# Second batch's probabilities transposed once: GpSimd adds the two blocks of a head, two triangles of ones part them again

## What is computed

```python
keep = (pos[None, :] < 4) | ((rel >= 0) & (rel < 128))   # rel = query - key
scores = np.where(keep, q @ k.T / 8, -1e9)
a = softmax(scores)
x = (a @ v) with the heads side by side                  # (2, 768, 512)
# mixer 1: low-rank token mixing (rank 32), then 512 -> 2048 -> 512
u = x + (x.T @ U @ V).T;           x = u + relu(u @ w1) @ w2
# mixer 2: 768 -> 256 -> 768 over the tokens, then 512 -> 1536 -> 512
u = x + (relu(x.T @ t1) @ t2).T;   out = u + relu(u @ w1) @ w2
```

## Time and profile before

| | us |
|---|---|
| median of three runs | 650.76 |
| profiled execution | 652.52 |
| its span | 650.7 |
| TensorE busy, matmuls | 632.9 |
| VectorE / ScalarE / GpSimd busy | 337.0 / 318.3 / 370.1 |

### The profile page before, as it was taken

One profiled execution on the slowest core, in us unless ns is written; L12 is line 12 of the kernel. 1 busy time (PEld: TensorE's weight loads), 2 busy tenths in 40 slices (PEclk: granted clock), 3 DMA queues, 4 the chain that ended last, 5 costly groups with the idle time before them and its releaser, 6 DMA issues.

```text
span 650.7 us, 10398 instructions
## 1 busy us (share of the span) xinstructions
PE 632.9 (97%) x3554; PEld 568.0 (87%) x3554; DVE 337.0 (52%) x720; ACT 318.3 (49%) x723; POOL 370.1 (57%) x371
## 2 busy tenths in 40 slices
PE   8999899999999999999999999999999999999997
PEld 6889698988989997999999988899998888899986
DVE  7776543332333422657576652297568226675411
ACT  5667644545544453745445444555445446344321
POOL 8545445655646473475757563585756446657262
PEclk9999989999999999999999999999999999999999
DMA  7434144342334242233222333233233343421142
GB/s 174 109 80 129 37 128 118 99 126 81 98 92 152 69 130 80 81 96 114 77 102 81 114 93 101 83 112 113 67 114 98 102 141 98 131 97 34 49 141 86
DMA packets 88420, 65.51 MB, mean 101 GB/s; under 512 B 43024, under 2 KB 72464, under 8 KB 88368
## 3 DMA queue, kind: packets, MB, share of 16 engines
q1 hardware_dynamic: 88368, 64.85, 35.1%
HBM read 61.42 MB, written 3.15 MB: 99 GB/s over the span
## 4 chain that ended last, share of the span: by engine, by line
PE 87%; DVE 5%; issue 3%; ACT 3%; POOL 1%; DMA 0%; DVEq 0%; ACTq 0%; POOLq 0%
PE bank L1400 34%; PE bank L1190 22%; PE bank L1366 10%; PE bank L1256 4%; PE bank L1227 4%; PE bank L1330 3%; PE bank L1293 3%; PE bank L1235 2%; PE bank L1307 2%; PE bank L1210 1%; PE bank L1274 1%; DVE masked L984 1%; PE bank L1392 1%; POOL w_lo L770 1%; DVE k_hi L962 1%
## 5 line engine op out<-in xcount | busy, mean ns | idle before, releaser
L770 POOL TENSOR_TENSOR w_lo<-w_raw,w_hi 128x512 fp32r<-128x512 f32 (+1 forms) x158 | 208.9, 1329 | 158.2 <-ACT w_hi L791 157.8
L791 ACT ACTIVATE w_hi<-w_raw 128x512 fp32r<-128x512 f32 (+1 forms) x158 | 96.5, 618 | 60.9 <-PE bank L1400 42.2
L1190 PE MATMUL bank<-b_hi,a_hi 128*128 128x384 f32 x280 | 94.6, 338 | 1.5 <-DVE temps L1096 1.5
L1190 PE MATMUL bank<-b_lo,a_hi 128*128 128x384 f32 x280 | 94.8, 339 | 0.0
L1400 PE MATMUL bank<-w_hi,hid_hi 128*128 128x512 f32 x216 | 87.6, 405 | 0.0
L1400 PE MATMUL bank<-w_hi,hid_lo 128*128 128x512 f32 x216 | 85.1, 394 | 0.0
L1400 PE MATMUL bank<-w_lo,hid_hi 128*128 128x512 f32 x216 | 84.7, 392 | 0.0
L823 ACT ACTIVATE probs<-masked,neg_max 128x264 f32<-128x264 f32 x96 | 49.5, 516 | 64.8 <-DVE neg_max L984 64.4
L1400 PE MATMUL bank<-w_hi,y_hid 128*128 128x512 f32 x216 | 71.1, 395 | 0.2
L984 DVE CUSTOM_DVE_ANT_0 masked<-bank,masks 128x264 f32<-128x264 f32 x96 | 41.1, 430 | 46.2 <-PE bank L1227 43.0
L735 POOL COPY p_sink<-probs 128x12 f32<-128x12 f32 x96 | 19.4, 204 | 72.1 <-ACT probs L823 70.7
(11 more groups left out here) (143 smaller groups left out, 1418.1 us busy)
## 6 DMA issues: line engine op xcount, KB each, us to landing
w_raw<-in_moe_w_ch_dram SPq DMA_DIRECT2D x144, 256.0 KB, 2.7
w_raw<-in_moe_w_ch_dram SPq DMA_DIRECT2D x20, 512.0 KB, 3.5
q_nat<-in_q_dram SPq DMA_DIRECT2D x12, 256.0 KB, 3.0
k_nat<-in_k_dram SPq DMA_DIRECT2D x12, 256.0 KB, 3.6
v_nat<-in_v_dram SPq DMA_DIRECT2D x12, 256.0 KB, 4.0
out_dram<-o_stage SPq DMA_DIRECT2D x11, 256.0 KB, 3.3
w_raw<-in_moe_w_tok_dram SPq DMA_DIRECT2D x6, 256.0 KB, 2.7
w_raw<-in_moe_w_tok_dram SPq DMA_DIRECT2D x8, 192.0 KB, 2.3
```

The lines of the kernel that those rows point to most:

```text
L770: nc.gpsimd.tensor_tensor(w_lo[:, split % NW, 0:n], w_raw[:, split % NR, 0:n], w_hi[:, split % NW, 0:n].bitcast(f32), ALU.subtract) \
L791: nc.scalar.activation(w_hi[:, split % NW, 0:n], w_raw[:, split % NR, 0:n], ACT.Copy) \
L1190: last = mm(bank[:, 0:HALF], w[at % 2][:, a, k, :], u[:, b_part, k, :], start=(first and n == 0), stop=(n == 5), skip_group_check=True)
```

## The change

For T = 7 to 11, the tiles of the second batch with two blocks: GpSimd adds the previous block's probabilities onto the own block's (one 128x128 sum for each head, ahead of its sink copy), TensorE waits for that sum and transposes it once, and VectorE, for all heads, multiplies the transposed sum from PSUM by two triangles of ones (key <= query, key > query) into the two halves of `probs_T`. The products with v stay. The triangles are built once by GpSimd in a part of `o_stage`, at the step `pv` of u = 8.

```diff
+        triangles = o_stage[:, 2, 0:2 * P].rearrange("p (a b) -> p a b", a=2)
...
         def blocks(T):
+            if T > NQ:
+                return [(0, T), (0, T - 1)]
...
+        def two_triangles(T):
+            return T > NQ
+
         def by_act(u):
-            return u % 2 == 1
+            return u % 2 == 1 and not two_triangles(u // H)
+
+        def act_copies(u):
+            return sum(by_act(v) for v in range(u + 1))
...
             elif by_act(at):
-                eng.wait_ge(probsT_by_act, (at + 1) // 2)
+                eng.wait_ge(probsT_by_act, act_copies(at))
             else:
-                eng.wait_ge(probsT_by_dve, at + 1 - (at + 1) // 2)
+                eng.wait_ge(probsT_by_dve, at + 1 - act_copies(at))
... (GpSimd)
                     copied += 1
+                    if two_triangles(T):
+                        pool.wait_ge(probs_ready, u + 1)
+                        nc.gpsimd.tensor_tensor(probs[:, u % 4, 0:P], probs[:, u % 4, 0:P],
+                                                probs[:, u % 4, BLK:BLK + P], ALU.add).then_inc(blocks_added, 1)
...
+                elif s == ("pv", H):
+                    nc.gpsimd.memset(triangles[:, :, :], 1.0).then_inc(triangles_built, 1)
+                    pool.wait_ge(triangles_built, 1)
+                    for n, step in enumerate((1, -1)):
+                        part = triangles[:, n, :]
+                        nc.gpsimd.affine_select(out=part, in_=part, compare_op=ALU.is_ge, fill=0.0, base=-n,
+                                                pattern=[[step, P]], channel_multiplier=-step) \
+                          .then_inc(triangles_built, 1)
... (VectorE)
-                    nc.vector.tensor_copy(probs_T[:, u % 2, 0:n], tp_banks[tp_bank_of[s]][:, 0:n]) \
-                      .then_inc(probsT_by_dve, 1)
+                    transposed = tp_banks[tp_bank_of[s]]
+                    if two_triangles(u // H):
+                        dve.wait_ge(triangles_built, 3)
+                        nc.vector.tensor_tensor(probs_T[:, u % 2, :].rearrange("p (a b) -> p a b", a=2),
+                                                transposed[:, 0:P].unsqueeze(1).broadcast_to([P, 2, P]),
+                                                triangles[:, :, :], ALU.mult).then_inc(probsT_by_dve, 1)
+                    else:
+                        nc.vector.tensor_copy(probs_T[:, u % 2, 0:n], transposed[:, 0:n]).then_inc(probsT_by_dve, 1)
... (TensorE)
                     tp_free(s)
-                    for j, (col, _) in enumerate(blocks(u // H)):
+                    if two_triangles(u // H):
+                        pe.wait_ge(blocks_added, u - (NQ + 1) * H + 1)
+                    for j, (col, _) in enumerate(blocks(u // H)[0:1 if two_triangles(u // H) else 2]):
```

More of the change, by code:

```diff
@@ L390, in attention_then_two_mixers @@
         masks_built = sem("masks_built")
+        triangles_built = sem("triangles_built")
+        blocks_added = sem("blocks_added")
         khi_zeroed = sem("khi_zeroed")
```

## The result

The changed kernel took 647.44 us (median of four, 646.91 to 648.74) against 650.78 us: a ratio of 0.9951, 95% interval 0.9938 to 0.9964, so 0.49% faster where 0.57% was forecast. A second set of runs gave 647.18 us, 0.9945 (0.9932 to 0.9958). Among the experiments, one execution of e5 was disturbed (1575 us) and is left out of its ratio.

The account below looks back on a forecast made before the run. TensorE, busy 97% of the 650.7 us span, was taken to bound the kernel. Savings of 32 x 0.11 + 4 x 0.04 + 4 x 0 = 3.7 us off the 650.76 us median gave 647.1 us, range 645.9 to 649.0.

Parts of the forecast that it names:

- The transposes, on the path: Units of T = 7 to 11: one transpose less on TensorE saves 0.11 us, in 32 units.
- Four sink stalls swallow the gain: Last heads of T = 7 to 10: the sink transpose waits for VectorE's masking, so these four units win nothing.
- Four units out of a stall earn 0.04 us: Units whose transposes start after a stall, three behind q's drain, one behind k: 0.04 us won each.
- GpSimd's sum and its queue: zero: Forty added 128x128 sums on GpSimd, 0.53 us each, and the work queued behind them cost TensorE nothing.
- GpSimd sets the pace: Rival, 7%: adds stretched to 1.5 us fill GpSimd's time per unit; gain gone, about 650.7 us.
- Part of the gain: Rival, 7%: adds arrive late in 12 of 40 units where GpSimd also splits q or k; 648.4 us.
- The added wait costs TensorE: Rival, 8%: a third wait before each of 40 transposes costs 0.15 us, 6.0 us in all; slower, 653.1 us.
- VectorE's multiply: zero: Copy out of PSUM as a 128x256 multiply, 0.43 us, one SBUF input: no collision with GpSimd, no cost.
- The triangles: zero: GpSimd's memset and two affine_selects behind the sink copy at 24.4 us: 1.4 us of work, covered, no cost.

Follow-up runs that it names:

- e5: Changed kernel with two spare GpSimd sums ahead of the real one in each of the 40 units; 652.34 us, ratio 1.0012.
- e1: Kernel before plus GpSimd's sum, written to a spare place, and TensorE's wait for it, still two transposes; 650.88 us, ratio 0.9998.
- e2: Kernel before with VectorE making all copies of transposed probabilities for T = 7 to 11; 650.93 us, ratio 1.0001.
- e3: Changed kernel without GpSimd's sum and TensorE's wait, so the output omits the previous block's probabilities; 647.61 us, ratio 0.9948.
- e8: Changed kernel with the sink transpose issued after six matmuls of the following mixer piece, T = 6 to 10; 642.77 us, ratio 0.9874.
- e9: Kernel before, two transposes kept, with the sink transpose issued inside the following mixer piece; 646.81 us, ratio 0.9935.

## Why the prediction was right

- *The transposes, on the path.* Forecast 0.11 us a unit, read from T = 6. Right: away from the stalls the units gained 0.09 to 0.13 us each (one, u = 64, only 0.03), and e1, e2 and e3 leave nothing else that could have made the gain.
- *Four sink stalls swallow the gain.* Right: the spacing of 1.01 us there did not move, and e8 against e9 gives the missing 0.46 us back once the stalls are gone.
- *Four units out of a stall earn 0.04 us.* Right behind the transpose (0.13 for 0.16), but incomplete: the stalls themselves became shorter, by 0.04 to 0.05 us each (0.59 for 0.63 at q's drain), which the forecast didn't have. That makes 0.2 us in all, and the sum came out at 3.7 partly because the other units gained a little less than 0.11 on average.
- *GpSimd's sum and its queue: zero.* Right; e1 shows it. The size was 0.48 where 0.53 was taken.
- *GpSimd sets the pace*, the rival, with 650.7 us from sums of 1.5 us. The real sum took 0.48, so it did not come about. e5 tried its price: three sums, 1.4 us of work, gave the kernel before's time within 0.2%. The number was right, and GpSimd's average room was indeed nearly gone. But TensorE did not wait in every unit: two thirds of the loss fell on the single unit in which GpSimd is late anyway.
- *Part of the gain*, the rival of 648.4 us with sums late in 12 units: TensorE waited for none of the sums.
- *The added wait costs TensorE*, the slower rival: excluded by e1.
- *VectorE's multiply: zero*, 0.42 us with one SBUF input beside GpSimd's work, 414 to 425 ns over all 40, and 414 to 426 in e5, where GpSimd is busy 95% of the time. Right. The rule cited from the Trainium skill, GPSIMD Engine Reference, Key points, is borne out: one SBUF input, no collision.
- *The triangles: zero.* Right: up to T = 6 both profiles keep step.
- The median fell by 3.3 us where 3.7 were forecast, within its interval; the stretch and the profiled pair, which have less noise, say 3.7 and 3.8.

## What to carry to other kernels

A unit of the kernel that already does what the edit will do elsewhere (here T = 6) prices the edit better than any duration: the spacing said 0.11 us where the duration said 0.28. Count such a saving only in units whose end TensorE sets itself; just before a wait for another engine it is worth nothing, until that wait is gone. And the room for added work on a helper engine is the room at its worst place in the queue, not its average idle time: one more sum in each unit already cost 0.4 us there while 16.6 us of waiting were left elsewhere.

## What was not expected of the hardware

**A dip of the clock, and a late start.** Executions of the kernel before differ by up to 1.9 us. The stretch tables from 81 to 86 us, the changed kernel first and then its second profile:

```profile
81.00:86.00 5.00, 4.74 (x24) 4.61 (x25) 2.20 (x7) 2.10 (x7) 1.41 (x2) 0.66 1.10 272
```
```profile
81.00:86.00 5.00, 4.69 (x33) 4.56 (x34) 3.60 (x11) 2.43 (x8) 1.42 (x2) 1.00 1.09 277
```

The granted clock is 0.66 in one and 1.00 in the other, a fall to the lower of its two levels (1.2 for 2.4 GHz) for most of it; twelve transposes take 2.77 us in one and 1.47 in the other, and everything behind comes 1.5 us later. In front of it TensorE was busy for only 2.6 of 4 us (77 to 81), in both. The first profile of the kernel before has the dip too, so that pair compares fairly, but medians mix executions with and without it.

There is a second source. In the profile of e3 no clock is lowered between 77 and 87 us, and yet its T = 7 begins 1.3 us later than in the second profile of the changed kernel. The difference is there from the first score product on (that second profile first, then e3):

```profile
7.16 0.60 PE L1241 MATMUL bank<-ident,q_nat 128*128 128x128 f32 x4
...
8.61 0.36 PE L1258 MATMUL bank<-k_hi,q_hi 128*128 128x264 f32 x1 [0.41 <-DVE k_lo L510]
```
```profile
8.32 1.06 PE L1237 MATMUL bank<-ident,q_nat 128*128 128x128 f32 x4
...
9.89 0.57 PE L1254 MATMUL bank<-k_hi,q_hi 128*128 128x264 f32 x1
```

Both lie before the edit does anything. Why TensorE is slower there for longer is open.

**One sum and one wait more, a shorter stall.** At q's drain the transpose starts 0.58 to 0.60 us after the product with v in the kernels in which GpSimd makes its sum in time and a third, long satisfied wait for it stands before the transpose, and 0.63 to 0.64 us in those without (the kernel before, e2, e3, e9). The timelines of e1, with two transposes, and e3, with one:

```profile
126.38 0.55 PE L1266 MATMUL bank<-v_nat,probs_T 128*128 128x64 f32 x4
...
126.97 0.41 PE L1245 MATMUL bank<-ident,probs 128*128 128x128 f32 x2
```
```profile
127.30 0.55 PE L1283 MATMUL bank<-v_nat,probs_T 128*128 128x64 f32 x4
...
127.93 0.30 PE L1262 MATMUL bank<-ident,probs 128*128 128x128 f32 x1
```

Three such stalls lie in the stretch, about half of e3's 0.26 us. e2 shows that it isn't ScalarE's relief. The runs have the sum and the wait for it either both or neither, so which of the two makes the release quicker, and why, is open.
